# Softmax over tokens kept beside attention, with fourteen expert weight buffers

## The reference

```
attention (B=4, H=8, S=768, D=48): for every t, complex decay a_t of length at most 0.999
    S_t = a_t[:, None] * S_(t-1) + k_t v_t^T          (complex state; k v^T is real)
    y_t = q_t . Re(S_t)
x = y as [3072 tokens, 384]
soft MoE: logits = x @ phi                             (32 columns = 8 experts x 4 slots)
    dispatch = softmax of logits over the 3072 tokens;  slot_in = dispatch^T @ x
    slot_out[e] = relu(slot_in[e] @ w1[e]) @ w2[e]     (8 experts, 384 -> 1024 -> 384)
    combine = softmax of logits over the 32 slots;      x2 = combine @ slot_out
MLP: h = relu(x2 @ w_in);  out = (h*h) @ w_out          (384 -> 2048 -> 384)
```

## Time and profile before

| | us |
|---|---|
| median of 3 runs | 725.77 (722.49 to 729.34) |
| profiled execution | 724.86 |
| its span | 723.1 |
| TensorE busy | 550.6 (76%) |
| VectorE busy | 400.6 (55%) |
| ScalarE busy | 303.0 (42%) |
| GpSimd busy | 155.9 (22%) |

### The profile page before, as it was taken

How to read it: one execution, slowest core, us unless ns; L and a number is a source line. 1 busy time by engine, 2 the same in 40 slices (tenths; PEclk the granted TensorE clock), 3 DMA queues, 4 the chain that set the end, 5 groups by cost and what they waited for, 6 DMA issues and landing times.

```text
span 723.1 us, 10760 instructions
## 1 busy us (share of the span) xinstructions
PE 550.6 (76%) x4152; PEld 403.4 (56%) x4152; DVE 400.6 (55%) x655; ACT 303.0 (42%) x485; POOL 155.9 (22%) x129
## 2 busy tenths in 40 slices
PE   1000029797579956999898977689999999999997
PEld 1000006575457735666687733236888888888885
DVE  1599986999699969997342142024233323333321
ACT  5775135271564524221222213215555555555553
POOL 4001000100001000100000001604555555555552
PEclk9555559899899998999898999899999999999999
DMA  6120091643756264697995699910010101000011
GB/s 232 50 81 0 16 243 30 140 99 90 239 133 148 59 142 111 194 251 196 262 287 117 224 405 420 427 53 0 1 45 0 45 1 43 1 22 22 2 44 44
DMA packets 46147, 88.97 MB, mean 123 GB/s; under 512 B 7568, under 2 KB 35344, under 8 KB 43792
## 3 DMA queue, kind: packets, MB, share of 16 engines
q1 hardware_dynamic: 39328, 67.05, 31.7%
q10 hardware_dynamic: 6768, 21.24, 8.8%
HBM read 59.83 MB, written 9.44 MB: 96 GB/s over the span
## 4 chain that ended last, share of the span: by engine, by line
PE 49%; DVE 19%; DMA 14%; SPq 6%; ACT 5%; issue 4%; POOL 1%; ACTq 0%; DVEq 0%; POOLq 0%
PE ps L1126 9%; PE ps L1125 9%; PE ps L1127 9%; DMA stk<-xout 9%; PE ps L918 6%; SPq L231 5%; DMA wt<-in_w 4%; PE ps L1109 3%; PE ps L904 3%; DVE tt L622 2%; DVE xout L718 2%; DVE big L627 2%; DVE tt L624 2%; SPq L241 2%; PE ps L1097 1%
## 5 line engine op out<-in xcount | busy, mean ns | idle before, releaser
L904 PE MATMUL ps<-ident 128*32 128x512 bf16 x297 | 85.1, 399 | 90.6 <-DMA stk<-xout 90.6
L569 POOL TENSOR_TENSOR hlo<-qs,hhi 128x512 fp32r<-128x512 f32 x96 | 123.9, 1291 | 127.8 <-DVE qs L887 126.8
L887 DVE TENSOR_TENSOR qs<-rs 128x512 f32<-128x512 f32 x96 | 67.2, 701 | 151.1 <-ACT rs L503 151.1
L918 PE MATMUL ps<-stk 112*128 112x224 f32 (+1 forms) x384 | 91.2, 402 | 45.8 <-DMA stk<-xout 38.2
L1126 PE MATMUL ps<-hlo,who 128*128 128x512 f32 x288 | 114.9, 399 | 0.0
L1125 PE MATMUL ps<-hhi,who 128*128 128x512 f32 x288 | 113.7, 395 | 0.4 <-POOL hlo L569 0.4
L918 PEld LDWEIGHTS ps<-stk 112*128 112x128 f32 x384 | 80.3, 229 | 59.7 <-DMA stk<-xout 45.5
L1127 PE MATMUL ps<-hhi,wlo 128*128 128x512 f32 x288 | 112.0, 389 | 0.0
L503 ACT ACTIVATE rs<-ps 128x512 f32<-128x512 f32 x96 | 57.3, 597 | 96.4 <-PE ps L1109 95.8
L904 PEld LDWEIGHTS ps<-ident 128*32 128x32 bf16 x297 | 23.1, 98 | 124.7 <-DMA stk<-xout 90.9
L546 POOL MEMSET big<- 128x2304 f32 x4 | 8.2, 2040 | 285.7 <-DVE big L627 285.7
(11 more groups left out here) (140 smaller groups left out, 779.5 us busy)
## 6 DMA issues: line engine op xcount, KB each, us to landing
stk<-xout SPq DMA_DIRECT2D x144, 128.0 KB, 3.8
wt<-in_w SPq DMA_DIRECT2D x10, 1536.0 KB, 16.9
xq<-in_xq SPq DMA_DIRECT2D x24, 384.0 KB, 4.7
wt<-in_w ACTq DMA_DIRECT2D x6, 1536.0 KB, 10.5
big<-in_a_all ACTq DMA_DIRECT2D x9, 768.0 KB, 6.5
vr<-in_v_all SPq DMA_DIRECT2D x24, 192.0 KB, 4.4
x_scratch<-xsb ACTq DMA_DIRECT2D x24, 192.0 KB, 3.7
xs<-x_scratch SPq DMA_DIRECT2D x4, 1152.0 KB, 7.7
```

Source lines behind the costliest of these rows:

```text
L569: pool.tensor_tensor(hlo[:, i % NHS, :], qs[:, i % NQS, :], hhi[:, i % NHS, :].bitcast(F32), ALU.subtract).then_inc(lo_ready, 1)
L887: dve.tensor_tensor(qs[:, i % NQS, :], rs[:, i % NQS, :], rs[:, i % NQS, :], ALU.mult).then_inc(sq_ready, 1)
L904: nc.tensor.matmul(ps[0:SL, bank, :], idb[:, 0:SL], idle, start=True, stop=True)
L918: last = nc.tensor.matmul(ps[:, h // 2, h % 2 * SK:h % 2 * SK + cols], x[:, 0:CH], x[:, CH:CH + cols], start=True, stop=True)
```

## The change

The softmax over tokens is made chunk by chunk while attention runs. For each chunk, logits are computed transposed (64 rows: 32 slots twice), copied with a minus sign (`copy_raw`), and VectorE keeps a running minimum of them (`running_max`). ScalarE takes the exponentials against the current extreme and, for the sums so far, the factor by which the extreme moved (`exponentials`, `rescale`, `scale_diag`). TensorE transposes the exponentials (`flip`), ScalarE copies them (`copy_flipped`), and two matmuls give the chunk's weighted sum of x with its weight, and the rescaled sums so far (`weighted_sums`), which ScalarE copies to `sums` (`copy_sums`). This runs four chunks behind the scores, so the loops have two more turns at the end. x isn't stored to DRAM nor read back. The idle matmuls are fewer in most turns. The sum over four groups (`sel`) and other constants are made at the start (18 in place of 12). `kts` has one buffer in place of two. The expert weights have 14 buffers in place of 8: 0 to 5 are loaded as before, 6 to 8 after the last keys and queries, 10 and 9 after the last stack, 11 to 13 after the last output, 14, 15 and w_in after the first slot outputs, w_out after the second. `cst` lies on weight 8, `who` on 6 and 7, `wlo` on w_out itself. Four pairs of experts go in the order 0, 1, 2, combine transposes 0 to 3, 3.

```diff
 C_SUB, C_READY = 4, 12
-NCONST = 12
+NCONST = 18
...
 @block.sync
-            for k in range(6, 8):
+            sp.wait_ge(kq_ready, 2 * NT)
+            for k in range(6, 9):
+                load_w(k)
+            sp.wait_ge(stacked[(NT - 1) % NST], 96 * ((NT - 1) // NST + 1))
+            for k in (10, 9):
                 load_w(k)
             sp.wait_ge(y_done, NT)
...
+            for k in range(11, NW):
+                load_w(k)
+            sp.wait_ge(o_done, 1)
+            for k in range(NW, 2 * NX):
+                load_w(k)
             sp.dma_start(wins[:], w_in).then_inc(ld_win, 16)
+            sp.wait_ge(o_done, 2)
             sp.dma_start(wouts[:], w_out).then_inc(ld_wout, 16)
-            for k in (8, 10, 9, 11, 12, 14, 13, 15):
-                load_w(k)
...
 @block.scalar
+            def copy_raw(m):
+                act.wait_ge(lgt_done, m + 1)
+                if m >= 2:
+                    act.wait_ge(flipped, m - 1)
+                nc.scalar.activation(eb[0:2 * SL, m % 2, 0:CH], lgt_ps, ACT.Copy, scale=-1.0).then_inc(raw_copied, 1)
+            def exponentials(m):
+                act.wait_ge(max_ready, m + 1)
+                e = eb[0:SL, m % 2, 0:CH]
+                nc.scalar.activation(e, e, ACT.Exp, scale=-1.0, bias=least(m)[0:SL]).then_inc(exp_done, 1)
+                if m:
+                    if m >= 2:
+                        act.wait_ge(sums_done, m - 1)
+                    nc.scalar.activation(rescale[0:2 * SL, m % 2:m % 2 + 1], least(m - 1), ACT.Exp, scale=-1.0,
+                                         bias=least(m)).then_inc(rescale_ready, 1)
+                    act.wait_ge(rescale_ready, m)
+                    nc.scalar.activation(scale_diag[0:2 * SL, m % 2, :], sel[0:2 * SL, :], ACT.Copy,
+                                         scale=rescale[0:2 * SL, m % 2:m % 2 + 1]).then_inc(diag_ready, 1)
...
+                    if 4 <= n:
+                        exponentials(n - 4)
                     if 0 <= n < NT and has_turn(n):
                         copy_kt(n, 0)
                         copy_kt(n, 1)
+                    if 4 <= n:
+                        copy_flipped(n - 4)
                     if 1 <= n <= NT:
                         copy_y(n - 1)
                     if 0 <= n < NT and has_turn(n):
                         copy_state(n)
-                    if 2 <= n < NT + 2:
-                        copy_lg(n - 2)
+                    if n == NT + 1:
+                        copy_raw(n - 2)
+                    if 4 <= n:
+                        copy_sums(n - 4)
+                    if 2 <= n <= NT + 1:
                         copy_x(n - 2)
-                        store_x(n - 2)
+                    if 2 <= n <= NT:
+                        copy_raw(n - 2)
...
             relu_h(0)
             relu_h(1)
+            relu_h(2)
             for b in range(4):
                 copy_c(b)
-                split_w(b)
-            relu_h(2)
+            relu_h(3)
             copy_c(4)
             copy_c(5)
-            relu_h(3)
+            for b in range(4):
+                split_w(b)
...
 @block.vector
                     if p < B:
                         parts_in(p, lo, mid)
+                    if 4 <= n:
+                        running_max(n - 4)
                     if 1 <= n <= NT:
                         apply_mask(n - 1, 0)
                         apply_mask(n - 1, 1)
...
+            dve.wait_ge(et_copied, NT)
+            step(dve.tensor_reduce(cm[:, 0, :], neg_lg, AX_X, ALU.min))
+            cmb = bass.AP(cm, cm[:, 0, :].offset, [list(cm[:, 0, :].ap[0]), [1, NT], [0, SL]])
+            step(dve.tensor_tensor(cexp[:], neg_lg, cmb, ALU.subtract), False)
...
 @block.tensor
+            def weighted_sums(m):
+                pe.wait_ge(et_copied, m + 1)
+                pe.wait_ge(x_copied, m + 1)
+                if m:
+                    pe.wait_ge(diag_ready, m)
+                    pe.wait_ge(sums_copied, m)
+                nc.tensor.matmul(sums_ps[0:SL], lgx[:, m % 2, :], xsb[:, m % 2, :], start=True, stop=True)
+                nc.tensor.matmul(sums_ps[SL:2 * SL], scale_diag[0:2 * SL, m % 2, :] if m else sel[0:2 * SL, :], sums[0:2 * SL, :],
+                                 start=True, stop=True).then_inc(sums_done, 1)
...
-            for n in range(NT + 2):
+            for n in range(NT + 4):
                 full = n < NT - NC
                 if n < NT:
-                    keep_busy(7 if full else 2)
+                    keep_busy(6 if full else 2)
                     scores(n)
+                if n == NT + 1:
+                    logits(n - 2)
+                if 4 <= n:
+                    flip(n - 4)
                 if 1 <= n <= NT:
-                    keep_busy(2 if full else 1)
+                    keep_busy(1)
                     outputs(n - 1)
                 if n < NT and has_turn(n):
                     keep_busy(2 if full else 1)
                     next_state(n)
-                if 2 <= n:
-                    keep_busy(2 if full else 1)
+                if 4 <= n:
+                    keep_busy(1)
+                    weighted_sums(n - 4)
+                if 2 <= n <= NT + 1:
+                    keep_busy(1)
                     turn_x(n - 2)
+                if 2 <= n <= NT:
+                    logits(n - 2)
...
-            keep_busy(10)
-            pe.wait_ge(soft_act, 1)
...
+            keep_busy(3)
+            pe.wait_ge(sums_copied, NT)
+            for k in range(KM):
+                nc.tensor.matmul(ps[:, 4, k * SL:(k + 1) * SL], sums[0:2 * SL, k * P:(k + 1) * P], sel[0:2 * SL, :], start=True,
+                                 stop=True)
```

More of the change, by code:

```diff
@@ L40, with program @@
 TT = B * S // TW
-def program(nc, a_all, xq_all, v_all, phi, w1, w2, w_in, w_out, x_dram, out):
+def program(nc, a_all, xq_all, v_all, phi, w1, w2, w_in, w_out, out):
     with ExitStack() as ctx:
@@ L114, in program @@
[L114 to L120 removed]
+        phs = place("phs", [P, NU, 2 * SL])
@@ new lines, in program @@
+        DX = DM + 1
+        xsb = place("xsb", [P, 2, DX])
+        eb = place("eb", [P, 2, CH + 1])
+        scale_diag = place("scale_diag", [P, 2, SL])
+        rescale = place("rescale", [P, 2])
+        attention_end = at[0]
+        after_at = SIZE // 32 * 32 - 4 * (P + SL + (DX + 31) // 32 * 32 + (2 + NT) * SL)
+        assert attention_end <= after_at, (attention_end, after_at)
+        at[0] = after_at
+        ident = place("ident", [P, P])
+        sel = place("sel", [P, SL])
+        sums = place("sums", [P, DX])
@@ L121, in program, with least @@
+        lgx = place("lgx", [P, 2 + NT, SL])
+        neg_lg = lgx[:, 2:]
+        def least(m):
+            return eb[0:2 * SL, (m + 1) % 2, CH:CH + 1]
+        NW = 14
+        wt = [place(f"wt{k}", [P, KM * FE], offset=k % NW * WT) for k in range(2 * NX)]
+        at[0] = NW * WT
+        sinz = place("sinz", [P, KM, NX, SL])
+        c4 = place("c4", [P, NT, 4, SL], F32R)
         cexp = place("cexp", [P, NT, SL])
         cm = place("cm", [P, 3, NT])
-        dm = place("dm", [P, 4, SL])
-        dg = place("dg", [P, SL])
@@ L418, in _ @@
             for p in range(B + 1):
-                for c in range(NC + 2 * (p == B)):
+                for c in range(NC + 4 * (p == B)):
                     n = (p - 1) * NC + c
@@ L539, in _ @@
             const(pool.memset(gst[R1 // 2:R1], 0.0))
-            const(pool.memset(xsb[:], 0.0))
+            const(pool.memset(xsb[:, :, 0:DM], 0.0))
+            const(pool.memset(xsb[:, :, DM:DX], 1.0))
+            const(pool.memset(sums[:], 0.0))
+            const(pool.memset(eb[:, 0, CH:CH + 1], 3.0e38))
+            const(pool.tensor_tensor(sel[:], ident[:, 0:SL], ident[:, SL:2 * SL], ALU.add))
+            for g in range(2, P // SL):
+                const(pool.tensor_tensor(sel[:], sel[:], ident[:, g * SL:(g + 1) * SL], ALU.add))
             assert made[0] == NCONST
@@ L803, in _ @@
                             scaled_mag(p + 1, t)
+            for m in range(NT - 3, NT):
+                running_max(m)
             done = [0]
@@ L898, in _, with keep_busy @@
             idle = bass.AP(idb.tensor, idb.offset, [list(idb.ap[0]), [0, 2], [1, 2 * P]])
-            def keep_busy(count, bank=7):
+            def keep_busy(count):
                 for _ in range(count):
-                    nc.tensor.matmul(ps[0:SL, bank, :], idb[:, 0:SL], idle, start=True, stop=True)
+                    nc.tensor.matmul(ps[P - SL:P, 7, :], idb[:, 0:SL], idle, start=True, stop=True)
             def scores(n):
@@ L961, in outputs, with logits @@
                 last.then_inc(y_done, 1)
+            def logits(m):
+                pe.wait_ge(y_copied, m + 1)
+                pe.wait_ge(s_copied, turns(min(m + 3, NT)))
+                if m:
+                    pe.wait_ge(raw_copied, m)
+                else:
+                    pe.wait_ge(ld_phi, 16)
+                for u in range(NU):
```

(12 more changed lines are left out.)

218 lines of the change are left out of this document (82 added, 136 removed).

## The result

The kernel after takes 720.41 us (median of 20 runs, 717.94 to 726.79), the kernel before 725.05 (median of 20, 721.77 to 730.48): ratio 0.9948, 95% interval 0.9926 to 0.9970. By the medians that is 4.6 us faster (3.8 by the ratio, 2.2 to 5.4 by its interval) where 11.6 were forecast, inside the range of 704 to 724 but near its upper end, and within the 1% that I had called no change.

A forecast was written before the change was run, and what follows sets the result against it. It took VectorE to bound attention's middle, TensorE its last batch, and traffic the softmax and experts; the MLP was carried over. Terms summed to -11.6 us from 724.86, 713.3, stated as 713.5 us, range 704 to 724.

The forecast's parts named there:

- edit 1: Softmax beside attention, no way through DRAM: last output matmul to first expert 12.2 us where it was 19.9, -7.7 us.
- Edit 2: Fourteen weight buffers: the 27.59 us expert-weight wait goes, first expert to first w_out product 52.4 us for 62.5, -10.1 us.
- H: The start of the first expert, from which the prediction counted the times of the experts and of w_out.
- rival B: Gain halved by a long pipeline rest after attention, late w_out, or both: 719 to 723 us; 0.20 together with Rival C.
- Rival C: Early weights not in when the experts start, 3.7 us each, 721 us for two; 0.20 together with rival B.
- The wait of VectorE's copy behind the combine weights: In the experts, first slot outputs start at H+9.0 where they stood at H+6.9: 2.1 us given back.
- Edit 3: What is added to attention, in several terms: start, minima, exponentials, TensorE's steps, batch borders and the stores that go.
- (a): At the start, six more constants on GpSimd hold up the first squares: +1.7 us, fully on the path.
- (b): In attention, one VectorE minimum for each chunk, 0.25 us, counted in chunks 4 to 17: +3.5 us.
- (c): In attention, ScalarE's exponentials ahead of the key copies delay three chunks, 0.7 us each, with table loads: +1.7 us.
- (d): TensorE's flip, sums and logits less idle matmuls: +1.8 us in the last batch; batch borders -1.0.
- Rival A: Attention eats the gain through queue order on ScalarE and VectorE: 34 us added, 18 us slower, 743 us; chance 0.12.

The follow-up runs named there:

- e12: Kernel after with the weighted sums and their copies left out for chunks 0 to 13 only; 717.79 us, ratio to before 0.9891.
- e5: Kernel after with two more idle matmuls ahead of each flip and each pair of sums behind the last chunk; 720.28 us, ratio to before 0.9942.
- e2: Kernel after with only the weighted sums and the copy of the sums left out for chunks 0 to 19; 711.77 us, ratio to before 0.9825.
- e6: Kernel after with weights 8 to 13 loaded late, as with eight buffers; 738.95 us, ratio to before 1.0169.
- e4: Kernel after with w_out loaded in four quarters with a semaphore each; 715.96 us, ratio to before 0.9882.
- e8: Kernel after with late constants (e3), w_out in quarters (e4) and idle matmuls behind the last chunk (e5) together; 712.79 us, ratio to before 0.9826.
- e10: e8 with VectorE's first copy of transposed rows put ahead of its last four steps on the combine weights; 711.75 us, ratio to before 0.9811.
- e3: Kernel after with the engines waiting for the six new constants only at the fifth chunk; 718.67 us, ratio to before 0.9920.
- e1: Kernel after with minimum, exponentials, flip, weighted sums and their copies left out for chunks 0 to 19; 713.57 us, ratio to before 0.9844.
- e9: Kernel after with two idle matmuls fewer in every turn from the fifth to the last chunk; 722.86 us, ratio to before 0.9944.
- e14: Kernel after with w_out and its low parts moved 32 bytes, to an odd multiple of 32 bytes; 725.43 us, ratio to before 1.0005.
- e13: Kernel before with the tile of w_out and its low parts moved 32 bytes, to a multiple of 64; 724.55 us, ratio to before 0.9981.

## Why the prediction was wrong

Counted against the medians: -11.6 were forecast and -4.6 came. Three rows of the table above are firm, and the first follows as the rest: +0.2 behind the last chunk (the mean of five such profiles is 20.4 us, that of four of before 20.2), -7.7 for the experts (55.4 against the mean of 63.1 in four of before), -3.4 for the MLP. That leaves +6.3 for attention, by the medians. The profiles alone would say +9.7, most of which excess is the 3.2 us by which the profiled executions of after stand above their medians. Against the forecast the four differ by +7.9, +2.4, -3.4 and +0.1 us, 7.0 in all.

- **The step that failed is edit 1's walk from the last output to the first expert.** Forecast 12.2 us and -7.7, measured 20.4 and about 0. With the clock at 1.00 it takes 16.9 (e12), so some 4.7 us lie in mis-sized terms and 3.5 in the clock. Two terms were mis-sized. A pair of sums was set at 0.5 us from 1.51/6, but the row it came from had four products side by side in different rows of the result; here each stands alone and takes 0.76 to 0.83 us even at full clock, the pair 1.6. The logits with phi as the weights were set at 0.45, as two products, and took 1.03: the kernel makes them in four. That it is the company of other products that makes the one row cheap is my reading of the code; no run tried it. And the walk counted the clock as full, where it fell to 0.53 between flip, copy and sums. Idle matmuls there give 3.5 us of it back in the profile (e5), but the clock also held without them in e2 and e12 (4 us), so what makes it fall stays open. The last turns, which I put at 2.9 and 2.1 us, took 3.2 with the clock up and 4.4 without.
- **Edit 2 held, and its warning came true.** The wait for weights went, and e6 shows what the early weights are worth. The experts' own steps were right within 1 us once GpSimd was out of the way (51.6 in e4, 52.4 forecast). The text had said that GpSimd's low parts were less than 1 us from being the bound. I had their start at H+36 + 1.5, where it came at H+39.5, and left out that GpSimd makes the first hidden low part only behind all four, and that TensorE then starts cold: +3.8 and +2.3 us in the profiles (e4: 4.8 us in all by the ratio). This is rival B, which came in both its halves, the long walk and the late w_out, and 720.4 lies in its 719 to 723. It had been given 0.20 together with C, and the low parts should have been in the sum.
- **The wait of VectorE's copy behind the combine weights** was forecast as 2.1 us given back. In the kernel after part of it was hidden, as the first experts ran at the lower clock (1.22 us idle at 454.11). It came out as 2.83 us idle and 1.7 us of lower clock when the way to it was made shorter (e5, e8), and fell to 0.94 us with e10.
- **Edit 3 came out right in sum (+6.2 forecast, +6.3 by the medians), but its parts aren't shown to be right.** (a) +1.8 for 1.7, by the first squares and, in e3, the first keys. (b), (c) the minima at 3.5 us and the exponentials ahead of the keys at 1.7: e1 against e2 leaves 3 to 4 us for both, within an uncertainty as large. (d) TensorE in the last batch, 1.8 forecast net of what it saves: the six sums alone are 4.8 between e12 and e2, and e9 gives nothing back for fewer idle matmuls. The table loads: one more, as forecast (14 in after, 13 before). The load at 221.40 us in after starts 0.02 us after the activation before it ends, and the next activation follows it at 222.70. So the row's price of 1.28 us held here too, against the drain that the Trainium skill's page "ScalarE: Activation LUTs", section "What ACT_TABLE_LOAD costs", adds to it.
- **The MLP "carried over as it is" was wrong by 5.7 us,** in the favourable direction, and that was luck. With the odd address back (e14) the change measures 1.0005: no gain at all. The place of a buffer was part of the diff, and no row could have priced it.
- Rival A, that attention eats the gain, didn't come: 6 us and not 34. Rival C didn't either; no expert waited for a weight in the profile of after.

## What to carry to other kernels

Before a price is taken from a row of small matmuls, look whether they ran side by side in the array; one that stands alone in a chain cost three times as much here (0.76 for 0.25 us), and a chain that makes TensorE wait between small products can also lose the clock. When a long wait is removed, list everything that used to lie under it and put the smallest margin into the sum: here GpSimd's low parts, VectorE's combine weights and a cold start each took back 1 to 4 us, and only when all were moved (w_out in quarters, one copy ahead, sums on the engine that is idle there) did the kernel reach 703.7 us, 3% below before. After a change of memory layout, compare the interval of the steady loop that "wasn't touched".

## What the runs showed of the hardware

- With TensorE at full clock, products of 128x128 by 512 columns in fp32 came every 0.2267 us, and every 0.235 us where the next load of weights read a tile on an odd multiple of 32 bytes (after and e14). The product behind it took 0.232 us. In the kernel before 0.2327 us in the mean, and 0.2314 with that tile on a multiple of 64 (e13), so the address isn't all of it.
- After 4.2 us without work TensorE started at the lower clock (granted 0.50), 0.63 us a product for 0.39, and ran so for about 5 us (2.3 us lost, after against e4); after 2.8 us too (4.48 for 2.79 us, e8).
- With four extra idle matmuls in each turn behind the last chunk the clock stayed at 1.00 through waits of 0.3 us (e5), where it fell to 0.53 in after, with waits of 0.86 us and without them. In e2 and e12 it stayed at 1.00 through the same waits of 0.86 us, also without them.
